# Transposing softmax probabilities in two row halves of TensorE's array, with the scores of a triple packed into three PSUM banks

## The reference

```python
# attention: batch 2, 8 heads, 768 positions, 64 features a head
scores = (q @ k.T) / sqrt(64) + bias          # bias: -slope(head) * distance
keep = (column < n_global) | (0 <= row - column < n_local)     # 8 and 96
a = exp(where(keep, scores, -1e9) - rowmax);  a = a / (sum(a) + 1e-9)
x = (a @ v)                                   # (2, 768, 8*64)
# gated FFN: h = relu(x @ w_in);  out = (h * sigmoid(conv3(h))) @ w_out
# spatial gating unit: h = relu(.. @ w_in); u, v = halves; v normalised,
#   mixed over positions with w_spatial, plus b_spatial; (u * v) @ w_out
```

## Time and profile before

| | |
|---|---|
| median of three runs | 361.47 us |
| the profiled execution, its own time | 361.26 us |
| its span, from the first to the last instruction | 359.5 us |
| PE busy | 351.6 us, 98% of the span |
| PE's weight loads (PEld) busy | 321.8 us |
| DVE, ACT, POOL busy | 215.7, 177.7, 89.2 us |
| one weight load: of a block to be turned, of `f1` (mean) | 140 ns, 188 ns |
| one matmul: of a turned block, of scores, of `f1` (mean) | 279, 300, 344 ns |
| share of PE in the chain that ended last | 92% |
| triples 4 to 15, the stretch that the change touches | 28.92 to 122.48 us |

### The profile page before, as it was taken

One profiled execution on the slowest core, in us unless ns is written; L12 is line 12 of the kernel. 1 busy time (PEld: TensorE's weight loads), 2 busy tenths in 40 slices (PEclk: granted clock), 3 DMA queues, 4 the chain that ended last, 5 costly groups with the idle time before them and its releaser, 6 DMA issues.

```text
span 359.5 us, 7397 instructions
## 1 busy us (share of the span) xinstructions
PE 351.6 (98%) x2891; PEld 321.8 (90%) x2891; DVE 215.7 (60%) x572; ACT 177.7 (49%) x451; POOL 89.2 (25%) x165
## 2 busy tenths in 40 slices
PE   7889999999999999999999999999999999999996
PEld 3558989998899999999889999998999999998885
DVE  6896898778776697789693942115853444441000
ACT  4887668776767688652464622114652111112112
POOL 4899796445554000000120300003400000000000
PEclk9999999999999999999999999999999999999999
DMA  7962342333314033302000000010341000001222
GB/s 215 400 238 67 97 122 83 123 129 113 112 46 162 2 117 119 116 19 100 0 2 1 2 0 0 2 43 2 119 133 45 0 0 2 0 2 60 106 100 94
DMA packets 12233, 27.77 MB, mean 77 GB/s; under 512 B 1568, under 2 KB 4256, under 8 KB 12192
## 3 DMA queue, kind: packets, MB, share of 16 engines
q1 hardware_dynamic: 11904, 27.10, 22.3%
q10 hardware_dynamic: 288, 0.13, 0.2%
HBM read 24.08 MB, written 3.15 MB: 76 GB/s over the span
## 4 chain that ended last, share of the span: by engine, by line
PE 92%; DVE 4%; DMA 1%; issue 1%; POOL 1%; ACT 0%; DVEq 0%
PE bank L1587 20%; PE bank L1589 20%; PE bank L1588 20%; PE bank L1543 19%; PE bank L1522 5%; PE bank L1498 5%; PE bank L1450 3%; DVE p_sb L1072 2%; DMA counts<-in_n_keys 1%; DVE denom L1081 0%; DVE xT L1094 0%; POOL p_sb L635 0%; ACT p_sb L735 0%; DVE table L1051 0%; DVE pt_sb L1089 0%
## 5 line engine op out<-in xcount | busy, mean ns | idle before, releaser
L1543 PE MATMUL bank<-xT,w_hi 128*128 128x384 f32 x256 | 69.5, 344 | 0.0
L635 POOL TENSOR_SCALAR p_sb<-p_sb,denom 128x256 f32<-128x256 f32 (+1 forms) x96 | 47.1, 508 | 38.2 <-DVE denom L1083 38.2
L735 ACT ACTIVATE p_sb<-p_sb,row_min 128x256 f32<-128x256 f32 (+1 forms) x96 | 46.3, 486 | 17.7 <-DVE row_min L1072 17.6
L1543 PEld LDWEIGHTS bank<-xT,w_hi 128*128 128x128 f32 x256 | 45.8, 188 | 0.3 <-issue 0.2
L1543 PE MATMUL bank<-xT,w_lo 128*128 128x384 f32 x128 | 44.0, 344 | 0.0
L1109 DVE SCALAR_TENSOR_TENSOR c_sb<-h_sb,conv_sb,c_sb 128x382 f32<-128x382 f32 (+1 forms) x64 | 42.6, 666 | 2.3
L1587 PE MATMUL bank<-g_hi,w_hi 128*128 128x386 f32 (+1 forms) x128 | 43.3, 338 | 0.0
L1589 PE MATMUL bank<-g_hi,w_lo 128*128 128x386 f32 (+1 forms) x128 | 43.2, 337 | 0.0
L1588 PE MATMUL bank<-g_lo,w_hi 128*128 128x386 f32 (+1 forms) x128 | 43.1, 337 | 0.0
L1072 DVE CUSTOM_DVE_ANT_0 p_sb<-bank,table 128x256 f32<-128x256 f32 (+1 forms) x96 | 33.0, 397 | 8.1 <-PE bank L1450 7.9
L656 POOL TENSOR_SCALAR rstd<-mean_var 128x1 f32<-128x1 f32 x12 | 4.7, 392 | 129.2 <-DVE mean_var L1137 129.2
(11 more groups left out here) (96 smaller groups left out, 784.1 us busy)
## 6 DMA issues: line engine op xcount, KB each, us to landing
stage<-in_weights SPq DMA_DIRECT2D x17, 512.0 KB, 3.3
v_sb<-in_v SPq DMA_DIRECT2D x8, 390.0 KB, 3.9
k_sb<-in_k SPq DMA_DIRECT2D x8, 384.0 KB, 4.2
out_dram<-out_sb SPq DMA_DIRECT2D x11, 256.0 KB, 2.0
q_sb<-in_q SPq DMA_DIRECT2D x13, 192.0 KB, 2.5
v_sb<-in_v SPq DMA_DIRECT2D x6, 260.0 KB, 3.7
k_sb<-in_k SPq DMA_DIRECT2D x5, 256.0 KB, 4.0
stage_late<-in_weights SPq DMA_DIRECT2D x2, 512.0 KB, 11.4
```

The lines of the kernel that those rows point to most:

```text
L635: nc.gpsimd.tensor_scalar(probs_h, probs_h, denom[:, u % SLOTS, h:h + 1], 1.0, ALU.mult, ALU.mult).then_inc(scaled, 1)
L735: nc.scalar.activation(p_sb[:, u % SLOTS, h, 0:n], p_sb[:, u % SLOTS, h, 0:n], ACT.Exp, bias=row_min[:, u % SLOTS, h:h + 1], scale=-1.0, a ...
L1543: last = nc.tensor.matmul(h_bank(j)[:, 0:C], w, x, start=r == 0, stop=r == F1_GROUP - 1)
```

## The change

- From triple 4 on each 128 by 128 block is turned as two matmuls: rows 0 to 63 of the block in the array's upper row half, rows 64 to 127 in its lower half. Each takes 64 rows by 128 columns as the stationary operand and moves a 64 by 64 identity. The two write to two adjacent PSUM banks (`turns`, banks 2 and 3). `weigh` reads the copied halves through a view with the halves as an extra dimension.
- PE's order in a triple from 4 on: turn units 0 and 1 in a row, twelve `f1`, the scores of triple `p` + 2, turn unit 2, twelve `f1`, weigh. Triples 0 to 3 keep their order, and the whole-block transposes.
- ACT copies units 0 and 1 with one instruction of 1024 columns (`copy_pair`) and the third with one of 512 (`copy_third`).
- The scores of triple 5 and later use three banks: 0 and 1 for unit 0, 0 and 5 for unit 1, 1 and 5 for unit 2. All of them wait for DVE to have read the whole triple before, and those of unit 2 also wait for PE's own unit 0 (`scored_one`), since another row half writes to bank 1 then.
- The orders of ACT and DVE are rewritten: `round_x` and `rest_of_x` come first in a triple; DVE's inversion comes after the first `taps`, and the biasing of triple `p` + 2 right behind it.

```diff
-                if p >= 2:
+                if p >= THREE_BANKS:
+                    pe.wait_ge(biased, 2 * TG * p)
+                elif p >= 2:
                     pe.wait_ge(biased, 2 * (TG * p - 1 if p > 2 else 2))
-                score_unit(u)
+                last = score_unit(u)
+                if p >= THREE_BANKS:
+                    last.then_inc(scored_one, 1)
...
-                wait_if(pe, biased, 2 * TG * p)
+                if p >= THREE_BANKS:
+                    pe.wait_ge(scored_one, p - THREE_BANKS + 1)
+                else:
+                    wait_if(pe, biased, 2 * TG * p)
                 score_unit(TG * p + 2).then_inc(scored, 1)
...
+            def turn_block(u, h, half, block):
+                rows = slice(half * HALF, (half + 1) * HALF)
+                at_col = turned_cols(u % TG).start + (2 * h + block) * HALF
+                return nc.tensor.transpose(turns[:, half, at_col:at_col + HALF],
+                                           p_sb[rows, u % SLOTS, h, block * P:(block + 1) * P], ident[rows, rows])
+
+            def turn_blocks(u):
+                p, tt = divmod(u, TG)
+                if tt == 0 and p > HP:
+                    pe.wait_ge(thirds_in, thirds(p - 1))
+                if tt == 2:
+                    pe.wait_ge(pairs_in, pairs(p))
+                for h in range(2):
+                    pe.wait_ge(scaled, 2 * u + h + 1)
+                    for block in range(keys(u) // P):
+                        turn_block(u, h, 0, block)
+                        last = turn_block(u, h, 1, block)
                 last.then_inc(turned, 1)
...
+            for p in range(HP, ALL_TRIPLES):
+                turn_blocks(TG * p)
+                turn_blocks(TG * p + 1)
+                for _ in range(F1_STEP // 2):
+                    f1(f1_next)
+                    f1_next += 1
                 if p + 2 < ALL_TRIPLES:
                     scores(p + 2)
+                turn_blocks(TG * p + 2)
+                for _ in range(F1_STEP // 2):
+                    f1(f1_next)
+                    f1_next += 1
                 for tt in range(TG):
                     weigh(TG * p + tt)
```

ACT's and DVE's orders for triples 4 to 15:

```diff
             for p in range(HP, ALL_TRIPLES):
-                u = TG * p
-                for tt in range(TG):
-                    if p + 1 < ALL_TRIPLES:
-                        soften(u + TG + tt)
-                    if tt == 2:
-                        relu_h(2 * (p - F1_FIRST))
-                    copy_pt(u + tt)
-                    if tt == 0:
-                        round_x(p - 1)
-                relu_h(2 * (p - F1_FIRST) + 1)
+                round_x(p - 1)
+                copy_pair(p)
+                if p == HP:
+                    soften(TG * (p + 1))
+                    soften(TG * (p + 1) + 1)
+                else:
+                    relu_h(2 * (p - F1_FIRST) - 1)
+                if p + 1 < ALL_TRIPLES:
+                    soften(TG * (p + 1) + 2)
+                relu_h(2 * (p - F1_FIRST))
+                copy_third(p)
+                if p + 2 < ALL_TRIPLES:
+                    soften(TG * (p + 2))
+                    soften(TG * (p + 2) + 1)
...
             for p in range(HP, ALL_TRIPLES + 1):
-                u = TG * p
-                for tt in range(TG):
-                    if p + 1 < ALL_TRIPLES:
-                        bias_scores(u + TG + tt)
+                if p == HP:
+                    bias_scores(TG * (p + 1))
+                    bias_scores(TG * (p + 1) + 1)
                 rest_of_x(p - 1)
...
                 if p > F1_FIRST:
                     taps(*divmod(2 * (p - 1 - F1_FIRST), KF))
                 if p + 1 < ALL_TRIPLES:
-                    invert_sums(u + TG, TG)
+                    invert_sums(TG * (p + 1), TG)
+                if p + 2 < ALL_TRIPLES:
+                    for tt in range(TG):
+                        bias_scores(TG * (p + 2) + tt)
```

More of the change, by code:

```diff
@@ L41 @@
 NEAR = WK + GK + PART
+HALF = P // 2
 GROUPS = 2 * B
@@ L252, in gen_vr, with psum @@
             return (gen_vr_a[:, 0, :], gen_vr_a[:, 1, :], gen_vr_b[:, 0, :])[j % VR]
-        banks = [ctx.enter_context(nc.psum_tensor(f"bank{i}", [P, 512], F32)) for i in range(8)]
+        def psum(name, shape):
+            return ctx.enter_context(nc.psum_tensor(name, shape, F32))
+        first_banks = [psum(f"bank{i}", [P, 512]) for i in range(2)]
+        turns = psum("turns", [P, 2, 512])
+        banks = first_banks + [turns[:, i, :] for i in range(2)] + [psum(f"bank{i}", [P, 512]) for i in range(4, 8)]
+        THREE_BANKS = HP + 1
         def score_cols(u, h):
             p, tt = divmod(u, TG)
-            bank = banks[(2, 5)[h] if tt == 2 else (6, 7)[h] if p == 1 else h]
-            at_col = tt % 2 * 2 * P
-            return bank[:, at_col:at_col + keys(u)]
+            if p >= THREE_BANKS:
+                bank, half = (((0, 0), (1, 0)), ((0, 1), (5, 0)), ((1, 1), (5, 1)))[tt][h]
+            else:
+                bank, half = (2, 5)[h] if tt == 2 else (6, 7)[h] if p == 1 else h, tt % 2
+            return banks[bank][:, half * 2 * P:half * 2 * P + keys(u)]
         def h_bank(j):
@@ L269, in pt_ps, with turned_cols @@
         def pt_ps(u):
[L270 to L276, removed]
+            bank = banks[(3, 4, 3)[u] if u < TG else (3, 6, 7)[u % TG]]
+            return bank[:, :].rearrange("p (h n) -> p h n", h=2)
+        def turned_cols(tt):
+            return slice(tt % 2 * 2 * P, (tt % 2 + 1) * 2 * P)
         xt_ps = banks[4]
@@ L310, in build_program @@
         pt_in_dve = sem("pt_in_dve")
+        pairs_in = sem("pairs_in")
+        thirds_in = sem("thirds_in")
         weighed = sem("weighed")
@@ L425, in wait_pt, with pairs, thirds @@
                 eng.wait_ge(pt_in, copies(u, False))
+        def pairs(p):
+            return p - HP + 1
+        def thirds(p):
+            return p - HP + 1
         def staged(n):
@@ L743, in copy_pt, with copy_pair, copy_third @@
                 nc.scalar.copy(pt_sb[:, u % PT_SLOTS, :, 0:n], pt_ps(u)[:, :, 0:n]).then_inc(pt_in, 1)
+            def copy_pair(p):
+                act.wait_ge(turned, TG * p + 2)
+                act.wait_ge(weighed, TG * p - 1)
+                nc.scalar.copy(pt_sb[:, 0:2, :, :], turns[:, :, :].rearrange("p f (s n) -> p s f n", s=2)
+                               ).then_inc(pairs_in, 1)
+            def copy_third(p):
+                act.wait_ge(turned, TG * p + 3)
+                act.wait_ge(weighed, TG * p)
+                nc.scalar.copy(pt_sb[:, 2, :, :], turns[:, :, turned_cols(2)]).then_inc(thirds_in, 1)
             def round_x(p):
@@ L1516, in weigh @@
                         pe.wait_ge(val_in[pg % 2], 16 * (pg // 2 - 1))
-                wait_pt(pe, u)
+                if g == 0:
+                    wait_pt(pe, u)
+                elif tt < 2:
+                    pe.wait_ge(pairs_in, pairs(pg))
+                else:
+                    pe.wait_ge(thirds_in, thirds(pg))
                 values = values_of(u)
@@ L1566, in _ @@
             f1_next = 0
-            for p in range(ALL_TRIPLES):
+            for p in range(HP):
                 for tt in range(TG):
@@ L1573, in _ @@
                         third_scores(1)
[L1574 to L1577, removed]
+                scores(p + 2)
+                for tt in range(TG):
+                    weigh(TG * p + tt)
+            for p in range(HP, ALL_TRIPLES):
[4 more added lines that the diff above has]
+                    f1_next += 1
                 if p + 2 < ALL_TRIPLES:
                     scores(p + 2)
+                turn_blocks(TG * p + 2)
+                for _ in range(F1_STEP // 2):
+                    f1(f1_next)
+                    f1_next += 1
                 for tt in range(TG):
```

16 lines of the change are left out of this document (12 added, 4 removed).

## The result

The changed kernel takes 362.59 us (median, 362.25 to 364.16), the kernel before 361.28 on the same chip: ratio 1.004, 95% interval 1.0026 to 1.0053. The profiled execution took 362.28 us. It is slower by 1.3 us, just under twice the 0.7 us that the prediction gave as what can be told from no change, and the interval excludes 1. The forecast was 362.0, within 360.7 to 364.5.

What follows compares the result with a forecast made beforehand. The prediction took PE's stream and its changes of shape to bound the kernel. Its terms, -6.9 + 6.6 + 0.5 + 0.2 - 0.2 + 0.3 = +0.5 us, gave 362.0 us against 361.47, range 360.7 to 364.5.

Steps and rivals of the forecast that it cites:

- The forecast's case: Whole kernel: six changes of shape take back what faster turning gives; 362.0 us, 360.8 to 363.4 by itself; chance 0.72.
- Turning, -6.9: PE from triple 4 on: 136 blocks turned as pairs of halves, 0.058 us each instead of 0.109, saving 6.9 us.
- Changes of shape, +6.6: PE, twelve triples: more switches of array shape between turning, `f1`, scores and weighing, 0.55 us a triple, adding 6.6 us.
- Rival two, no drain between halves and full array: PE: both changes between halves and `f1` are free, 4.8 us less, 357.2 us; chance 0.10.
- (a): Triple 3: all three units of triple 5's scores wait for DVE's read of unit 14; +0.5 us, once.
- (b): Third unit's scores wait for PE's own first unit: 0.02 us in eleven triples, +0.2 us; bounds 0 to 0.05 each.
- (c): Triple 4: its wait of 0.2 us for `rest_of_x(3)` goes, since DVE does that first; -0.2 us.
- (d): POOL scales unit 22 at 8.6 us after triple 6's start, PE wants it at 8.3: +0.3 us, bounds 0 and 0.6.
- the halves don't pay: Rival on PE's turning: the load paces a pair at 0.109 us, gaining 0 instead of -6.9; 368.9 us; chance 0.08.
- The late chain through POOL: Rival: ACT, DVE and POOL make turning late in every long triple, about 0.3 us each; +3, 365 us; chance 0.10.

Runs made afterwards that it cites:

- Experiment 4: Changed kernel, but only the first 32 rows of each half turned, halving moving columns, loads still 128 columns: 362.00 us, ratio 1.0017 to the kernel before.
- experiment 2: Changed kernel with six of the first twelve `f1` moved between the turning of units 0 and 1: 366.93 us, ratio 1.0161 to the kernel before.
- experiment 6: Changed kernel, but in triple 3 the first unit's scores of triple 5 wait as before, not for the whole biasing: 361.94 us.
- experiment 5: Kernel before, third unit's scores waiting for PE's own first unit from triple 6's scores on, DVE's wait moved ahead of all three units: 362.21 us, ratio 1.0026.
- experiment 1: Changed kernel with its order, banks and waits, but each block turned whole, 128 columns moving: 364.22 us, ratio 1.0082 to the kernel before.
- experiment 7: Changed kernel, but from triple 5 on all three units' blocks turned in a row, the third into banks 0 and 1: 362.69 us, ratio 1.0039.
- experiment 9: Kernel of experiment 8, but from triple 8 on all three units turned in a row, with `copy_third` ahead of `relu_h`: 360.73 us, ratio 0.9984.
- experiment 8: Kernel of experiment 6, with the heads of the first and third units' scores swapped: 361.91 us, ratio 1.0019 to the kernel before.

## Why the prediction came out as it did

The forecast's case happened: what the turning gained, the changes of shape took back, and waits made it a little slower. The time lies 0.6 us above the forecast, inside its range. As a difference it was 1.3 us, where 0.5 was forecast: the kernel before came out 0.2 us faster beside it than the 361.47 that the forecast started from. Term by term:

- **Turning, -6.9.** Right in kind, a tenth too large. A pair takes 0.0625 us, not 0.058: 136 x (0.109 - 0.0625) = -6.3. I had taken the gap between the first two loads of a row; with many in a row it is the gap between later ones. Experiment 4 shows that neither the moving columns nor the rows set it, which leaves the load.
- **Changes of shape, +6.6.** Right. 0.20 into `f1` is read off the timeline, and experiment 2 charges 0.36 for one into `f1` and one out of it, against 0.35. Rival two, no drain between halves and full array, is excluded: so is its bound of 0.
- **(a) Triple 3's scores, +0.5.** Right: +0.51 by the start of triple 4, and experiment 6 gives 0.44 of it back in its trace. What I wrote beside it, that without the shift POOL's unit 13 would cost 0.4, was wrong, a row of two units read as one. It changed nothing in the sum.
- **(b) PE waiting for itself, +0.2.** This is the mis-sized term, beyond even its upper bound of 0.05 a triple. I took the load to be free as soon as the matmul waited for has ended, which left 0.02 us a triple. But the load starts 0.12 to 0.13 us behind that end; the matmul with the signal is the last of its round, so that 0.36 and not 0.41 us lie between its start and the third unit's turn; and then the next round follows 0.160 behind the first instead of 0.136. That is 0.09 in eleven triples: +1.0, which experiment 5 measures by itself (ten triples, +1.0).
- **(c) `rest_of_x(3)`, -0.2.** Triple 4 is 0.14 shorter in all, though it now holds the self-wait of 0.09, so the wait has gone.
- **(d) POOL late, +0.3.** It came, but in triple 7's start alone: sixteen loads in 0.75 instead of 0.58 us, +0.17. Unit 22 was ready 8.6 us into triple 6, as I had put it; only its second head's blocks had to wait.

The sum of the terms as measured, -6.3 + 6.6 + 0.5 + 1.0 - 0.2 + 0.2, is +1.8; the two profiled executions differ by 1.0, the medians by 1.3. Some 0.4 us of the rest is `f1`: behind the first gap of each run its starts lie 0.1737 us apart on average, in two runs of twelve, and 0.1757 before, in three of eight; that is some 0.03 us a triple. I hadn't forecast that, and why it is so stays open. What remains is within the rounding of twelve times six changes. So part of the closeness is luck: the pair and the self-wait were put 1.4 us too low together, and `f1` and POOL gave back 0.5. A long triple takes 8.14 where I forecast 7.98. Of the 0.16, 12 x 0.0045 = 0.05 is the pair and 0.07 the self-wait; the rest is that I started from triple 7's 8.04, while triples 5, 12 and 13 took 8.09 to 8.10 before. The forecast's own bounds, 360.8 to 363.4, were added up loosely: by its terms the low end is 362.0 - 0.54 - 0.5 = 361.0. The range was cut wider and doesn't hang on it.

Of the rivals, "the halves don't pay" is excluded by the spacing and by experiment 1: by the rows a load of 64 rows and 128 columns takes the place of the 0.06 us gap seen before, not that of `f1`'s 0.11. The late chain through POOL turned up in one triple, not in all; experiment 7 shows how near it was, for the third unit due 2 us sooner cost some 1.5 us in triples 6 and 7 and nothing in triples 8 to 13.

## What to carry to other kernels

When a faster form of an operation has another array shape than its neighbours, count the borders before the blocks: here a border costs 0.14 to 0.20 us, and a block's gain was 0.047, so a group of eight blocks about pays for its two borders and one of four doesn't. The way on was to make the groups longer (experiment 9), and to check for each triple whether the engine that feeds the longer group has the time. And a wait of an engine on its own earlier work is not over at that work's end: price the signal's way back, and don't let two waits meet on one instruction of a stream that has no slack.

## What I had not expected of the hardware

- PE waiting on a semaphore of its own matmul: the load starts 0.12 to 0.13 us behind the matmul's end (96.548 to 96.674; 96.292 to 96.409 in experiment 8).
- A second wait on one load adds an instruction of 51 ns, and 0.09 us to the row (1.23 against 1.14).
- Loads of fp32 blocks to be turned follow one another 0.0625 us apart, with 64 rows and with 32, 128 columns each, and the matmuls' 64 or 32 columns don't matter. Those of `f1`, also 128 columns, take 0.11; the Trainium skill's 107 ns for 128 columns (TensorE: Matmul & The Clock Gate, section "LDWEIGHTS (loading the stationary operand)") fits only `f1`'s of the two.
- After 1.6 us in which PE had nothing to do in triple 3, two of the traces show about 3 us at half the clock, and others, with the same stand, don't; it costs 1.1 to 1.6 us when it comes, in 5 of 39 executions. After a stand of 0.8 to 1.1 us no trace here shows it.
